# Attention and two MoE layers on one core: later waits for the sink transposes, another order of two ScalarE copies, logits turned into rows by TensorE

## What is computed

```python
def _attn_ref(q, k, v, n_sink, window):            # (2, 8, 768, 64), 4, 128
    scores = scale * np.matmul(q, k.transpose(0, 1, 3, 2))
    keep = is_sink | in_window
    scores = np.where(keep, scores, -1000000000.0)
    scores = scores - np.max(scores, axis=-1, keepdims=True)
    a = np.exp(scores)
    a = a / (np.sum(a, axis=-1, keepdims=True) + 1e-09)
    return np.matmul(a, v).astype(np.float32)

def _moe_ref(x, w_a, w_b, w_out):                  # 1536 x 512, d_ff 1536
    return ((x @ w_a) * (x @ w_b) @ w_out).astype(np.float32)

def _moe2_ref(x, w_gate, w1, w2):                  # E = 8, F = 1024
    logits = x @ w_gate
    order = np.argsort(-logits.flatten())
    # each token goes to the first (token, expert) in this order whose expert has room
    for e in range(E):
        mask = assigned == e
        out[mask] = np.maximum(x[mask] @ w1[e], 0.0) @ w2[e]
```

## Time and profile before

| | us |
|---|---|
| median of 3 runs | 611.72 |
| lowest, highest | 611.55, 611.83 |
| the profiled execution | 611.83 |
| its span, first to last instruction | 610.0 |
| TensorE busy | 596.4 |
| VectorE busy | 416.6 |
| GpSimd busy | 322.3 |
| ScalarE busy | 289.8 |

### The profile page before, as it was taken

The page is one execution under the profiler, slowest core; times in us unless marked ns, Lnnn a source line. Parts: engine busy times, 40 slices in busy tenths (PEclk is TensorE's granted clock), DMA queues, the critical chain, the costliest instruction groups (busy, mean ns, idle before and its releaser), DMA issues.

```text
span 610.0 us, 13277 instructions
## 1 busy us (share of the span) xinstructions
PE 596.4 (98%) x4708; PEld 508.6 (83%) x4708; DVE 416.6 (68%) x1329; ACT 289.8 (48%) x692; POOL 322.3 (53%) x281
## 2 busy tenths in 40 slices
PE   8999999999999999999999999999999999999995
PEld 6777778999899899889977887777777889888894
DVE  4767661332256529998889998888957767677670
ACT  5999973332333333323322224243436765667540
POOL 8677663555455556545456662000086786667741
PEclk9999999999999999999999999999999999999999
DMA  9324291443663474465114151412569677877500
GB/s 275 118 85 155 84 329 46 123 119 105 174 173 115 128 208 139 121 166 163 38 37 155 54 190 35 157 53 94 200 229 387 211 234 252 302 262 256 165 26 27
DMA packets 85456, 94.40 MB, mean 155 GB/s; under 512 B 13808, under 2 KB 63248, under 8 KB 84752
## 3 DMA queue, kind: packets, MB, share of 16 engines
q1 hardware_dynamic: 83056, 86.86, 44.5%
q0 software_dynamic: 2048, 6.29, 3.2%
q10 hardware_dynamic: 288, 0.41, 0.2%
HBM read 87.20 MB, written 6.34 MB: 153 GB/s over the span
## 4 chain that ended last, share of the span: by engine, by line
PE 82%; DVE 13%; ACT 2%; issue 2%; DMA 0%; POOL 0%; DVEq 0%; ACTq 0%; POOLq 0%
PE bank L1419 14%; PE bank L1299 11%; PE bank L1301 11%; PE bank L1300 11%; PE bank L1518 8%; PE bank L1541 4%; PE bank L1236 4%; PE bank L1520 4%; PE bank L1286 4%; PE bank L1220 3%; DVE ge L948 2%; DVE ge L950 2%; PE bank L1312 2%; PE bank L1459 1%; DVE ge L966 1%
## 5 line engine op out<-in xcount | busy, mean ns | idle before, releaser
L548 POOL TENSOR_TENSOR wl_ab<-raw_ab,wh_ab 128x1024 fp32r<-128x1024 f32 x46 | 110.3, 2398 | 108.0 <-ACT wh_ab L663 108.0
L1299 PE MATMUL bank<-xh,wh_ab 128*128 128x384 f32 x384 | 130.6, 340 | 1.2 <-DVE hid L994 1.2
L1301 PE MATMUL bank<-xh,wl_ab 128*128 128x384 f32 x384 | 128.5, 335 | 0.0
L1300 PE MATMUL bank<-xl,wh_ab 128*128 128x384 f32 x384 | 128.4, 334 | 0.0
L663 ACT ACTIVATE wh_ab<-raw_ab 128x1024 fp32r<-128x1024 f32 x46 | 48.8, 1061 | 139.1 <-PE bank L1301 139.1
L619 POOL TENSOR_TENSOR w2l<-w_raw,w2h 128x1024 fp32r<-128x1024 f32 x32 | 75.7, 2390 | 35.9 <-DVE w1l L1105 35.7
L994 DVE TENSOR_TENSOR hid<-hid,bank 128x384 f32<-128x384 f32 x48 | 26.6, 553 | 82.9 <-ACT hid L679 82.9
L1299 PEld LDWEIGHTS bank<-xh,wh_ab 128*128 128x128 f32 x384 | 72.1, 188 | 7.9 <-issue 7.7
L1518 PE MATMUL bank<-xg,w1h 128*128 128x384 f32 x256 | 73.6, 359 | 0.8 <-issue 0.6
L1300 PEld LDWEIGHTS bank<-xl,wh_ab 128*128 128x128 f32 x384 | 72.1, 188 | 0.0
L1301 PEld LDWEIGHTS bank<-xh,wl_ab 128*128 128x128 f32 x384 | 72.1, 188 | 0.0
(11 more groups left out here) (166 smaller groups left out, 1220.7 us busy)
## 6 DMA issues: line engine op xcount, KB each, us to landing
w_sb<-in_moe_w_dram SPq DMA_DIRECT2D x8, 2048.0 KB, 8.4
w_raw<-in_moe_w_dram SPq DMA_DIRECT2D x32, 512.0 KB, 8.4
raw_ab<-in_moe_w_a_dram SPq DMA_DIRECT2D x48, 256.0 KB, 3.1
raw_ab<-in_moe_w_b_dram SPq DMA_DIRECT2D x48, 256.0 KB, 3.5
raw_out<-in_moe_w_out_dram SPq DMA_DIRECT2D x24, 256.0 KB, 2.7
lb<-logit_rows SPq DMA_DIRECT2D x4, 1536.0 KB, 6.4
v_sb<-in_v_dram SPq DMA_DIRECT2D x8, 384.0 KB
woT<-in_moe_w_outT_dram SPq DMA_DIRECT2D x1, 3072.0 KB, 11.7
```

Source lines behind the costliest of these rows:

```text
L548: pool.tensor_tensor(wl_ab[s % 2][:, :], raw_ab[s % 3][:, :], wh_ab[s % 2][:, :].bitcast(F32), ALU.subtract).then_inc(abl_done, 1)
L1299: pe.matmul(dst, lh, rh, start=first, stop=False)
L1300: pe.matmul(dst, lh, rl, start=False, stop=False)
L1301: return pe.matmul(dst, ll, rh, start=False, stop=last)
```

## The change

The sink transposes go to the banks of the second and fourth unit, and wait for the second and the fourth mask of the scores just issued (`2 * a + 2` for `a + 1`); the scores of the second and fourth unit, and no longer the first two, wait for the sinks to be copied out. The banks of the gated products and of the `w_out` products are renumbered to match. In `h_part` the copy of `hid` stands before the split. The nine DMAs into `L` go; instead TensorE transposes `LS_sb` in step 12c + 1 of the following pass (`logits(c - 1)`), and VectorE copies it out in step 12c + 2 (`l_copy`). Waits tie these to VectorE's use of the same bank, and VectorE's waits on its own last sum go. For expert 1, ScalarE splits the four quarters of w2 after f = 4, 5, 6, 7 of expert 0; before, it was the first two after f = 6 and 7, and the last two after `xg` and `w1h` of expert 1.

```diff
@@ -321,7 +321,6 @@
         wg_in, l_ready, l_out, y_stored, l_stored = (sem("wg_in"), sem("l_ready"), sem("l_out"),
                                                      sem("y_stored"), sem("l_stored"))
         lb_in = [sem(f"lb_in{c}") for c in range(NC)]
-        l_in = [sem(f"l_in{c}") for c in range(NC - 1)]
         routed = sem("routed")
         parts_cleared, ge_ready, ge_diag, ge_counted = (sem("parts_cleared"), sem("ge_ready"), sem("ge_diag"),
                                                         sem("ge_counted"))
@@ -343,13 +342,12 @@
 
 
         SB_, PT_, OB_ = banks[0:4], banks[4:6], banks[6:8]
-        SINKS = [SB_[i][0:2 * n_sink, MID:MID + P] for i in (0, 1)]
-
-        AB_, BB_ = (banks[2], banks[0]), (banks[3], banks[1])
-        LT_, LG, LATE = banks[4:6], banks[6], banks[7]
+        SINKS = [SB_[i][0:2 * n_sink, MID:MID + P] for i in (1, 3)]
+
+        AB_, BB_, LT_, LG, LATE = banks[0:2], banks[2:4], banks[4:6], banks[6], banks[7]
         LATER = LATE[:, P:P + C]
         OWN, WOG = LG[:, P:P + C], LG[:, 0:NF * E]
-        YB_ = [banks[i] for i in (2, 3, 0, 1, 5, 4)]
+        YB_ = [banks[i] for i in (0, 2, 1, 3, 5, 4)]
         CNT, POS = banks[6], banks[6]
         IDX = [banks[7][:, 0:2 * E], banks[6][:, P:P + 2 * E]]
         H2_, XG_, O2_ = banks[0:4], banks[4:6], banks[6:8]
@@ -441,11 +439,6 @@
                 sp.dma_start(lb[:, c, :, :].rearrange("p e t -> p (e t)"),
                              l_dram.rearrange("(c x) b -> c (x b)", c=NC)[c:c + 1, :].broadcast_to([P, E * C])
                              ).then_inc(lb_in[c], 16)
-                if c < NC - 1:
-                    for t in range(TC):
-                        sp.dma_start(L[:, TC * c + t, :],
-                                     l_dram.rearrange("(c x) b -> c (x b)", c=NC)[c, :].rearrange(
-                                         "(e t p) -> t p e", e=E, t=TC)[t], allow_slow_non_contiguous=True).then_inc(l_in[c], 16)
 
             half = FIRST_TILES
             sp.dma_start(q_sb[0][:, 0:half * P], qT[0, :, 0:half * P]).then_inc(q_first, 16)
@@ -674,9 +667,9 @@
                     act.wait_ge(s_masked, UNITS)
                 if s == 1:
                     act.wait_ge(xl_done, DUOS)
+                act.activation(hid[:, f, C * c:C * (c + 1)], AB_[s % 2][:, 0:C], ACT.Copy).then_inc(a_out, 1)
                 if s + 2 < STEPS:
                     split_ab(s + 2)
-                act.activation(hid[:, f, C * c:C * (c + 1)], AB_[s % 2][:, 0:C], ACT.Copy).then_inc(a_out, 1)
 
             half = FIRST_TILES
             act.dma_start(k_sb[0][:, 0:half, :], kT[0, :, 0:half, :]).then_inc(k_first, 16)
@@ -723,6 +716,7 @@
 
             def LS_copy(c):
                 act.wait_ge(ls_ready, 1)
+                act.wait_ge(l_ready, c)
                 act.wait_ge(l_stored, 16 * c)
                 act.activation(LS_sb[:, :], LT_[(c + 1) % 2][0:E, 0:C], ACT.Copy).then_inc(ls_out, 1)
 
@@ -814,17 +808,14 @@
                         act.wait_ge(h2l_done, KF * e)
                     act.activation(hT_rest[:, f, :], SUM_REST[n % 4], ACT.Relu).then_inc(h2r_done, 1)
                     act.activation(hTh[:, f, :], SUM[n % 4], ACT.Relu).then_inc(h2h_done, 1)
-                    if e == 0 and f >= KF - 2:
-                        high_w2(1, f - (KF - 2))
+                    if e == 0 and f >= KF - 4:
+                        high_w2(1, f - (KF - 4))
                     if f % 2 == 1 and 1 <= e < E - 1:
                         high_w2(e + 1, f // 2)
                 if e + 1 < E:
                     xg_high(e + 1)
                     for kk in range(KD):
                         high_w1(e + 1, kk)
-                if e == 0:
-                    high_w2(1, 2)
-                    high_w2(1, 3)
                 act.wait_ge(o_ready, e + 1)
                 if e >= 2:
                     act.wait_ge(o_stored[e % 2], 32 * (e // 2))
@@ -910,7 +901,6 @@
                 if i >= 1:
                     dve.wait_ge(wog_ready, i)
                 dve.tensor_tensor(gate_sum, gate_half[0:E, :], gate_half[TILE:TILE + E, :], ALU.add).then_inc(gate_summed, 1)
-                dve.wait_ge(gate_summed, i + 1)
 
             def logit_sums(c):
 
@@ -918,12 +908,12 @@
                 dve.tensor_tensor(LT_half[:, :], LT_sb[0:P // 2, :], LT_sb[P // 2:P, :], ALU.add).then_inc(LT_halved, 1)
                 dve.wait_ge(LT_halved, c + 1)
                 if c >= 1:
+                    dve.wait_ge(l_ready, c)
                     dve.wait_ge(l_stored, 16 * c)
                 dve.tensor_tensor(LS_sb[:, :], LT_half[0:E, :], LT_half[TILE:TILE + E, :], ALU.add).then_inc(ls_out, 1)
-                dve.wait_ge(ls_out, c + 1)
 
             def l_copy(c):
-                dve.wait_ge(l_ready, 1)
+                dve.wait_ge(l_ready, c + 1)
                 dve.tensor_copy(L[:, TC * c:TC * (c + 1), :],
                                 LG[:, 0:TC * E].rearrange("p (t e) -> p t e", t=TC)).then_inc(l_out, 1)
 
@@ -978,13 +968,15 @@
                     dve.wait_ge(mask_up, 1)
                     dve.wait_ge(later_up, 2)
                     dve.wait_ge(lb_in[c - 1], 16)
-                    dve.wait_ge(l_in[c - 1], 16 * TC)
+                    dve.wait_ge(l_out, c)
+                if s == 3 * NF + 2 and k == 0:
+                    dve.wait_ge(l_ready, c)
                 for unit in here[k:k + 1] if k < 2 else here[2:]:
                     sum_rows(*unit)
                 if c > 2 and F_COMPARE <= f < F_COMPARE + E:
                     if f == F_COMPARE and k == 0:
                         dve.wait_ge(lb_in[c - 1], 16)
-                        dve.wait_ge(l_in[c - 1], 16 * TC)
+                        dve.wait_ge(l_out, c)
                     compare(TC * (c - 1) + k, f - F_COMPARE)
 
             def h_part(s):
@@ -1014,11 +1006,13 @@
                     dve.wait_ge(gateT_out, len(GATE_AT))
                     dve.tensor_scalar(LATER[:, 0:P], before16[:, :], -1.0, None, ALU.mult).then_inc(later_up, 1)
                     dve.memset(LATER[:, P:C], -1.0).then_inc(later_up, 1)
+                if s % NF == 2 and s > NF:
+                    l_copy(s // NF - 1)
             compare_of_step(STEPS - 1, 0)
             compare_of_step(STEPS - 1, 1)
             compare_of_step(STEPS - 1, 2)
             l_copy(NC - 1)
-            dve.wait_ge(l_out, 1)
+            dve.wait_ge(l_out, NC)
 
             n = 0
 
@@ -1208,7 +1202,7 @@
                     pe.wait_ge(k_in[par], 16 * (p // 2 + 1))
                 if u >= 4:
                     pe.wait_ge(s_masked, u - 3)
-                if u % 4 < 2:
+                if u % 2 == 1:
                     pe.wait_ge(sinkT_out, sinks_before(max(0, u // 4 - 2)))
                 lo, n, ns = keys(i)
                 if ns:
@@ -1242,7 +1236,7 @@
                     return
                 pe.wait_ge(sinkT_out, sinks_before(q))
                 for a in range(2):
-                    pe.wait_ge(s_masked, min(4 * (q + 2) + a + 1, UNITS))
+                    pe.wait_ge(s_masked, min(4 * (q + 2) + 2 * a + 2, UNITS))
                     pe.transpose(SINKS[a], pn_sb[(2 * q + a) % 4][:, P:P + n_sink, :].rearrange("p k h -> p (k h)"),
                                  ident[:, :]).then_inc(sinkT_ready, 1)
 
@@ -1388,7 +1382,14 @@
             def logits(c):
 
                 pe.wait_ge(ls_out, c + 1)
-                pe.wait_ge(row_summed, ROWS)
+                if c == 0:
+                    pe.wait_ge(mask_up, 1)
+                else:
+                    pe.wait_ge(l_out, c)
+                if c == 1:
+                    pe.wait_ge(row_summed, 2 * TC * E)
+                if c == 2:
+                    pe.wait_ge(row_summed, ROWS - 4 * 4)
                 for t in range(TC):
                     mm = pe.transpose(LG[:, t * E:(t + 1) * E], LS_sb[:, t * P:(t + 1) * P], ident[0:E, 0:E])
                 mm.then_inc(l_ready, 1)
@@ -1435,6 +1436,8 @@
                 if s - 1 in GATE_AT:
                     gate_columns(GATE_AT.index(s - 1))
                 logit_part(s)
+                if f == 1 and c > 0:
+                    logits(c - 1)
             count_groups(STEPS - 2)
             y_products(3)
             logit_sums(NC - 1)
```

## The result

The changed kernel takes 618.25 us (median of four runs, 617.83 to 618.47) against 611.77 (611.55 to 611.83) for the kernel before, measured in turn with it: 1.0106 times as long, 95% interval 1.0089 to 1.0124, or 6.5 us more. The prediction said 619.7, with a range of 614.4 to 622.0. The profiled execution took 617.87 us, of which 616.1 are its span; the span of before was 610.0, so 6.1 us are to be found in the two traces.

A forecast was written before the change was run, and what follows sets the result against it. TensorE's own queue was taken to set the end almost everywhere. Sinks 5.3, first MoE 1.4 and expert 1 1.2 sum to 7.9; the span of 610.0 becomes 617.9, with 1.8 outside it 619.7 us, range 614.4 to 622.0.

The forecast's parts named there:

- Part 1: Attention, sink transposes: the second of a pair waits for the fourth mask, 14 pairs pay, 5.3 us in all.
- nothing heals it: Attention: the whole quad moves with the late transpose, and only a few tenths of already existing waits come back.
- Part 2: First MoE: copying hid first delays ScalarE's split, so GpSimd's low part comes late; 1.2 us before step 28.
- d: First MoE: loss each time the delayed split makes TensorE wait, once in two steps: 0.24 us.
- rival (b): First MoE: GpSimd's recorded spans are too long and the split has room: 617.5 us; chance 0.15.
- Parts 3 and 4: First MoE: VectorE's earlier hid gains 0.15 at 269 and 0.3 at the end; two groups of logit transposes cost 0.6.
- TensorE arrives 4 x 0.24 = 0.96 later: First MoE, third pass: late steps delay TensorE's arrival at the multiply that released it at 269.29 by 0.96 us.
- The last comparison: First MoE, end of last pass: VectorE's lead shortens TensorE's wait by about 0.3 us.
- Part 5: Start of expert 1: ScalarE waits for w2's quarters, xg starts 2.6 later, TensorE goes on 1.2 us later.
- (a): Attention: ScalarE sets the pace of a quad and the new wait hides in its shadow: 614.4 us; chance 0.12.
- (c): First MoE: VectorE's lead is what counts, 1.0 at 269.29 and 0.3 at the end, faster: 610.4 us; chance 0.08.
- (d): Whole kernel: new waits and VectorE's new lead cancel: 611.7 us; chance 0.05.

The follow-up runs named there:

- the sink part alone: Kernel before with only the sink banks (MoE banks renumbered) and the transposes' waits for the second and fourth mask changed: 616.31 us, ratio 1.0073.
- taken from step 28 on: Kernel before with ScalarE's copy of hid ahead of the split only from step 28 on: 610.64 us, ratio 0.9978.
- three quarters early: Kernel before with three quarters of w2 of expert 1, instead of two, split between the relus of expert 0: 611.84 us, ratio 1.0002.
- all four quarters late: Kernel before with all four quarters of w2 of expert 1 split after w1h: 611.82 us, ratio 1.0002.
- the kernel with both edits: Kernel before with the copy of hid first from step 28 on and all w2 of expert 1 split after w1h: 610.64 us, ratio 0.9982.

## Why the prediction was right, and where its sizes were off

**Part 1, 5.3 forecast, 4.3 on the trace, 4.5 alone.** Place, releaser and healing were stated; the first two hold. The waits before the second transpose are 0.51 to 0.54 in the seven wide quads (forecast 0.32 to 0.52) and 0.26 to 0.58 in six narrow ones, 6.1 in all; the first of the 14 pairs loses nothing. The step that failed is "nothing heals it": 0.10 a pair comes back in front of the value products, and 0.1 to 0.2 more in three of the narrow quads, at the start of the next scores. In all 1.8 is won back; the forecast had written off 0.3. Three quads take 10.9 us, not the 11.1 that were to be seen.

**Part 2, d = 0.24 forecast, 0.13 measured.** The chain is as described, with GpSimd's end 0.05 ahead of the load, which rules out rival (b), and the cost comes once in two steps. Mis-sized was d. I took it from the 0.30 by which the copy exceeds the spare, and from one late load (0.15 behind its beat, with 0.20 of waiting); but the load that waits has less behind it (0.10 in place of 0.17), in each of the two steps of a pair, and the two together lose 0.13. Taken by itself, the one late load of the kernel before would have given 0.15, nearly the size. Ahead of step 28 the late steps cost 0.65 against 1.2.
The Trainium skill (Perfetto Trace Analysis, section GPSIMD Engine Instruction) says to treat such spans as unreliable. For the ends of this subtract the trace speaks against it: 17 loads start 0.05 us behind a recorded end.

**Parts 3 and 4, the wait at 269.** It is gone, as forecast. The whole first MoE costs 0.89 where 1.4 was forecast. Ahead of step 28 the forecast had 1.2 + 0.6 = 1.8, and the trace has 1.62 (4.32 at the first steps, 5.94 at 225.44, the start of step 28): the late steps 0.65, the two groups of transposes 0.97. That the sums are this close is luck: the steps were priced 0.55 too high and the groups 0.37 too low. I had priced a group at the 0.28 of its loads, without the 0.25 of gap ahead of them. The row that I used does not show a gap; the weight loads of the kernel before do, at the same place (its timeline):

```profile
320.68 0.26 PEld L1393 LDWEIGHTS bank<-ident,LS_sb 8*128 8x128 f32 x3 [0.37 <-issue]
```

From step 28 on the forecast had -0.15, and the trace has -0.62 (5.32 at 274.58). The step that failed is "TensorE arrives 4 x 0.24 = 0.96 later": it lost 0.38 between 225.44 and 269.88, since d is 0.13, and since the kernel before loses about 0.14 itself around 248.84, which is not lost twice. The last comparison gave 0.14, not 0.3.

**Part 5, 1.2 forecast, 0.89 measured.** Landing, order and the shorter low parts came as described. The 0.3 too much add up from rows: the first low part starts at 466.33 in the time of before, not 466.5, the copies of `o_sb` follow after 2.28 and not 2.35, and the last low parts 0.79 behind them and not 0.85.

**Rivals.** (a) falls with the sink part alone. (b) falls with the loads behind GpSimd. (c) was right in its mechanism and wrong in its reach: the lead of VectorE is worth 1.0 at 269 when it is taken from step 28 on (1.11 less 0.15), and in the change it gives back no more than its late steps cost. (d), which needed both, did not occur. The forecast's 7.9 against 6.1 on the trace is 1.0 from the sinks, 0.5 from the MoE and 0.3 from expert 1, all to one side. The sinks and the late steps were priced at their waits, and not at their waits less what moves up behind them; the transposes erred the other way and hid part of it.

## What to carry to other kernels

Read behind a new wait as well as at it: what follows the waiting instruction often stood apart from it by a little, and takes up part of the delay. A lead given to an engine counts from the point where that engine last waited for the one you want to speed up, so an edit that pays in one stretch can be limited to it, and should be where it costs in the others. And when a step is moved off one collision, look one round further for the next one.

## What the runs showed of the hardware that I had not expected

VectorE and GpSimd on subtracts of SBUF tiles do not slow each other down a little: one of them stands. In expert 1 of the kernel before, VectorE's pair starts at 463.86, GpSimd's ends at 465.56, and 465.56 + 2.36 is 467.92, against a recorded end at 467.79; with three quarters early, 465.46 + 2.36 = 467.82 against 467.69. In these two places GpSimd was under way first and VectorE stood. When VectorE was under way first, GpSimd stood. With all four quarters late, VectorE's second pair is there first (timeline of that kernel):

```profile
465.82 2.35 DVE L1103 TENSOR_TENSOR w1l<-w_sb,w1h 128x1024 fp32r<-128x1024 f32 x2
```

and ends at 468.17; GpSimd's four parts, begun at 466.59, end at 477.48, and 468.17 + 4 x 2.36 is 477.61.
The Trainium skill (SBUF — State Buffer, section Who interferes with whom) says that a VectorE instruction with two SBUF inputs and a GpSimd instruction that reads SBUF exclude each other for a whole instruction, and that the one issued first wins. These traces agree. They add that VectorE, once under way, kept the place for both instructions of its pair (465.82 to 467.03 and 466.95 to 468.17), although GpSimd's first part has its recorded start inside the first of them; the kernel with both edits shows the same (VectorE's pair ends at 467.16, GpSimd's first part runs from 465.58 to 469.42).

Three small transposes between two streams of products cost a gap ahead of them beside the 0.28 us of their own loads: 0.25 at each of the three new places in the change, and 0.36 at the fourth, among the products with `w_out`, which the kernel before has too. In its waits view, weight loads:

```profile
PEld bank L1394 <- issue: 1.1, 4, 0.4
```

Why, no run here shows.
